# Four waits taken out of GpSimd's tap loop, and its rms step moved up two places

## The reference

```python
# 1. dynamic convolution, 8 heads of 24 features, 7 causal taps, weights by softmax over the taps
w = exp(weight_gen - max(weight_gen)); w = w / (sum(w) + 1e-9)
x1[b, s, h, g] = sum_k w[b, s, h, k] * x_pad[b, s + k, h, g]
# 2. a layer with a rational function, 192 -> 2048 -> 192
h = x1 @ w_in
P = a0 + a1*h + a2*h**2 + a3*h**3
Q = 1 + |b0|*|h| + |b1|*h**2
x2 = (P / (Q + 1e-6)) @ w_out
# 3. RMS norm and a gated layer, 192 -> 1536 -> 192
xn = x2 / sqrt(mean(x2**2) + 1e-6) * rms_g
out = (silu(xn @ w_gate) * (xn @ w_val)) @ w2_out
```

## The kernel before

| step | waits for | VectorE's step, with the iteration's blocks |
|---|---|---|
| mul 2 | `qy_ready` (blk - 2) * 8 + 7 | qy 6 of block i - 2 |
| add 2 | `py_ready` (blk - 2) * 8 + 8 | py 7 of block i - 2 |
| add 3 | `qy_ready` (blk - 1) * 8 + 1 | qy 0 of block i - 1 |
| add 4 | `act_ready` (blk - 1) * 8 + 2 | newton 1 of block i - 1 |

## Time and profile before

### The profile page before, as it was taken

The page is one execution under the profiler, slowest core; times in us unless marked ns, Lnnn a source line. Parts: engine busy times, 40 slices in busy tenths (PEclk is TensorE's granted clock), DMA queues, the critical chain, the costliest instruction groups (busy, mean ns, idle before and its releaser), DMA issues.

```text
span 1418.4 us, 21333 instructions
## 1 busy us (share of the span) xinstructions
PE 1390.6 (98%) x7488; PEld 1248.9 (88%) x7488; DVE 1164.8 (82%) x1520; ACT 1069.3 (75%) x1387; POOL 381.9 (27%) x273
## 2 busy tenths in 40 slices
PE   7879999999999999999999999999999999999998
PEld 6668989989898999889898988989989899898987
DVE  8899978888887888888888788888879788888621
ACT  4877878778788877878887787987878787777521
POOL 3332332404233141332413233240423324000000
PEclk9989999999999999999999999999999999999999
DMA  8201000000000001000000100000000000000000
GB/s 243 77 0 32 2 31 12 15 28 0 31 11 31 11 0 42 0 31 11 31 11 0 42 0 31 11 31 11 0 31 11 31 11 1 12 1 1 12 12 12
DMA packets 12517, 32.35 MB, mean 23 GB/s; under 512 B 1604, under 2 KB 7234, under 8 KB 12480
## 3 DMA queue, kind: packets, MB, share of 16 engines
q1 hardware_dynamic: 11744, 31.61, 6.9%
q10 hardware_dynamic: 736, 0.23, 0.1%
HBM read 25.55 MB, written 6.29 MB: 22 GB/s over the span
## 4 chain that ended last, share of the span: by engine, by line
PE 93%; DVE 4%; ACT 2%; issue 0%; DMA 0%; ACTq 0%; DVEq 0%
PE dn L752 40%; PE bank L743 10%; PE bank L744 10%; PE bank L745 10%; PE bank L746 10%; PE bank L747 10%; PE bank L759 2%; DVE num L681 1%; DVE num L668 1%; PE dn L828 1%; DVE num L665 1%; PE dn L822 1%; DVE den L676 0%; DVE num L687 0%; DVE den L666 0%
## 5 line engine op out<-in xcount | busy, mean ns | idle before, releaser
L752 PE MATMUL dn<-dn_w,num 128*128 128x192 f32 x2048 | 374.9, 327 | 5.4 <-DVE num L687 5.4
L752 PEld LDWEIGHTS dn<-dn_w,num 128*128 128x128 f32 x2048 | 340.5, 191 | 11.7 <-DVE num L687 6.2
L538 ACT ACTIVATE den<-bank,coef 128x512 f32<-128x512 f32 x256 | 175.7, 686 | 177.8 <-PE bank L747 169.8
L752 PE MATMUL dn<-dn_w,glu 128*128 128x192 f32 x1536 | 279.6, 326 | 0.0
L665 DVE TENSOR_TENSOR num<-num,bank 128x512 f32<-128x512 f32 x256 | 174.7, 682 | 111.1 <-ACT num L540 109.2
L752 PEld LDWEIGHTS dn<-dn_w,glu 128*128 128x128 f32 x1536 | 255.0, 190 | 4.0
L681 DVE SCALAR_TENSOR_TENSOR num<-num,coef,seed 128x1024 f32<-128x1024 f32 x128 | 165.9, 1297 | 57.1 <-ACT seed L557 56.6
L540 ACT ACTIVATE num<-bank,coef 128x512 f32<-128x512 f32 x256 | 199.9, 781 | 0.0
L666 DVE SCALAR_TENSOR_TENSOR den<-den,coef,bank 128x512 f32<-128x512 f32 x256 | 189.6, 741 | 0.0
L668 DVE SCALAR_TENSOR_TENSOR num<-num,coef,bank 128x512 f32<-128x512 f32 x256 | 189.6, 741 | 0.0
L712 DVE TENSOR_TENSOR glu<-glu,bank 128x512 f32<-128x512 f32 x192 | 130.8, 681 | 66.2 <-PE bank L747 64.9
(11 more groups left out here) (122 smaller groups left out, 2033.5 us busy)
## 6 DMA issues: line engine op xcount, KB each, us to landing
x_in<-in_x_dram SPq DMA_DIRECT2D x14, 960.0 KB
out_dram<-y_out SPq DMA_DIRECT2D x16, 384.0 KB, 2.3
w_blk<-in_weight_gen_dram SPq DMA_DIRECT2D x14, 112.0 KB, 2.0
dn_w<-in_moe_w_out_dram SPq DMA_DIRECT2D x1, 1536.0 KB, 9.8
dn_w<-in_moe_w_out_dram SPq DMA_DIRECT2D x1, 1152.0 KB, 17.8
num<-in_moe_w_in_dram SPq DMA_DIRECT2D x1, 768.0 KB, 6.3
num<-in_moe_w_in_dram SPq DMA_DIRECT2D x2, 384.0 KB, 7.9
x_in<-in_x_dram SPq DMA_DIRECT2D x1, 768.0 KB
```

The source lines that it names most:

```text
L538: act.activation(chunk(den, c % 8), h, ACT.Abs, scale=B_RAW[:, 1:2])
L752: done = pe.matmul(banks[:, j // 2, j % 2 * D:(j % 2 + 1) * D], acts[:, j * P:(j + 1) * P], w, start=first and j % 2 == 0, stop=last, skip ...
```

## The change

The function `while_reading_psum` and its two calls go, so that `mul 2`, `add 2`, `add 3` and `add 4` start as soon as their data and buffers are there. In GpSimd's program `rms 0 2` moves ahead of `add 3 0` and `mul 5 0`; it stood behind them.

```diff
 POOL_PROGRAM = program("""
-add 6 1, low 4 2, low 5 2, low 6 2, low 7 2, less 0 0, norm 0 0, mul 0 0, mul 1 0, mul 2 0, add 1 0, mul 3 0, add 2 0, mul 4 0, add 3 0, mul 5 0, rms 0 2,
-add 4 0, mul 6 0, add 5 0, low 0 1, low 1 1, low 2 1, low 3 1,
+add 6 1, low 4 2, low 5 2, low 6 2, low 7 2, less 0 0, norm 0 0, mul 0 0, mul 1 0, mul 2 0, add 1 0, mul 3 0, add 2 0, mul 4 0, rms 0 2, add 3 0,
+mul 5 0, add 4 0, mul 6 0, add 5 0, low 0 1, low 1 1, low 2 1, low 3 1,
 """)
...
-            def while_reading_psum(blk, step):
-
-                if step == ("mul", 2):
-                    wait(pool, qy_ready, (blk - 2) * 8 + 7)
-                elif step == ("add", 2):
-                    wait(pool, py_ready, (blk - 2) * 8 + 8)
-                elif step == ("add", 3):
-                    wait(pool, qy_ready, (blk - 1) * 8 + 1)
-                elif step == ("add", 4):
-                    wait(pool, act_ready, (blk - 1) * 8 + 2)
...
                 else:
-                    while_reading_psum(blk, ("mul", k))
                     if k >= 3:
...
             def tap_add(blk, k):
-                while_reading_psum(blk, ("add", k))
                 wait(pool, tap_ready, (blk - 1) * K + k + 1)
```

## The result

The changed kernel takes 1428.57 us (median of 5, 1427.53 to 1430.36), the kernel before 1420.38 us in the same comparison: the ratio is 1.0059, with a 95% interval of 1.0044 to 1.0074. It is slower by 8.2 us. The prediction was 1420.2 us, no change, with 1425.0 as the upper end of its range: it was wrong.

The account below looks back on a forecast made before the run. TensorE, never idle from 105.5 us on, was taken to bound the kernel. VectorE's 2.45 us lateness per iteration came from its own idle, so 0 us over 13 iterations: 1420.2 us forecast, range 1418.0 to 1425.0.

Parts of the forecast that it names:

- What bounds the kernel: TensorE, busy for 1308.50 of 1308.50 us from 105.5 us on, sets the pace; earlier GpSimd steps cannot shorten it.
- the first one of the walk: mul 2 in block 10's iteration: asks at 745.6, waits for two VectorE instructions, ends where the old wait put it; cost 0.
- the walk: Block 10's iteration priced step by step without the waits: VectorE loses about 2.45 us in two places, TensorE 0.
- the row at 116.76: Trace row in an early block: a GpSimd product waited for two L687 in a row, 3.87 us; both kept their time.
- the row at 107.61: Trace row: a GpSimd product met a running L681, took 2.16 us, and got in between two back-to-back L681.
- Both signs of being wrong: TensorE waits for L668, L697 or L712 after 105.5 us; or collisions lengthening more than three VectorE instructions per iteration.
- Rival 2: Two meetings add up ahead of up1 5: 0.41 us per iteration over its slack, 5.3 us slower, 1425.5 us; chance 0.05.
- add 2 and mul 4: Block 10: mul 4 runs 754.9 to 756.4, makes VectorE's L687 1.25 us late; up1 5 keeps 0.65 us; TensorE cost 0.
- rms and add 3: After rms at 776.57, add 3 loses to the first L687; the second ends 1.2 us late; no TensorE cost.
- rival 1: GpSimd wins its turns at 776 to 781: second L687 2.6 us late, up to 7.4 us slower; chance 0.10.
- the threshold of 2.80 us: VectorE lateness allowed at the L697/L665 pair: 2.53 us of idle plus 0.27 us of margin before TensorE loses time.

Follow-up runs that it names:

- The wait removed: The kernel before with only mul 2's wait on qy 6 removed, the other three waits and the old order kept: 1429.13 us, ratio 1.0062.
- the wait put back: The changed kernel with one of its four waits put back, that of mul 2 on qy 6: 1420.87 us, ratio 0.9999.
- the order-alone kernel: The kernel before with only the order changed, rms 0 2 ahead of add 3 and mul 5, all four waits kept: 1420.32 us, ratio 0.9997.
- The closed-pair kernel: The changed kernel with mul 2's wait on qy 6 put back and VectorE's glu 7 moved behind newton 1: 1463.73 us in one run.
- The run with `mul 2` behind `py`: The changed kernel with a wait put back for mul 2, on py 6 in place of qy 6: 1420.34 us, ratio 0.9999.
- the kernel of 1452.9 us: The kernel before with the waits of add 2, add 3 and add 4 removed, mul 2's wait and the old order kept: ratio 1.0233.

## Why the prediction was wrong

*What bounds the kernel* was right: TensorE sets the pace, no GpSimd step was on its path, and nothing was to be gained. Every kernel that was not slower came out within 0.1% of the one before.

*The step that failed* is the first one of the walk: "`mul 2` asks at 745.6, meets a running instruction and another behind it, as at 116.76, and comes out where the old wait had put it. Cost 0." In its place the runs show that `mul 2` goes straight on from `mul 1` and `py 6` waits, that `add 1` then gets in ahead of `qy 6`, and that VectorE loses 3.0 us, not 0. Even in iteration 3, where `mul 2` does wait for `py 6`, it gets in ahead of `qy 6`. The wait removed and the wait put back each move the whole of it. I had taken the row at 116.76, the only one of three in which GpSimd came off worst, for the rule, although the row at 107.61 showed GpSimd between two back-to-back steps. Where three rows disagree, each order should have been priced. (That product also ended 1.40 us behind the second L687, at 120.63 against 119.23, and not 1.54; nothing hangs on it.) Both signs of being wrong that the prediction named are there: TensorE waits for L712's result, and four VectorE instructions per iteration are lengthened, not at most three.

*The margin was not the one I looked at.* Rival 2 had the place and the first loss right ("if `mul 2` gets in ahead of the L681"), but it counted one collision of the two, 0.8 us of lateness, and asked only `up1 5` (1.93 us). The waiter that decided is `down2 2`: 752.89 - 751.25 = 1.64 us behind `glu 2`. With 2.2 us of lateness the excess is 0.6 us, and TensorE lost 0.61 + 0.10. Rival 2 had been given a chance of 0.05.

*add 2 and mul 4*: in the changed kernel they run ahead of `newton 6`, which keeps 1.2 us, because VectorE is late by then. With mul 2 held back (the kernel of 1420.87 us) `newton 6` takes 2.44 us against the 2.5 foreseen, and is covered, as foreseen.

*rms and add 3*: the order was rival 1's and not the walk's: `add 3` gets in ahead of `newton 0`, and `newton 1` is late by 2.4 us where rival 1 had 2.6. That this costs nothing was right, and the order-alone kernel shows it. But the threshold of 2.80 us at the next L665 was not the first one: `gate 9` waits for the `glu 7` between the newton steps. In the kernel before it starts at 780.33, with `glu 7` at 777.91 for 0.68 us, a margin of 1.74; the lateness there is 1.66. The closed-pair kernel, which puts `glu 7` behind a second held-up step, pays 43 us for missing it.

*The Trainium skill's rule* (SBUF — State Buffer, "Who interferes with whom": the first to issue holds the shared ports, the other blocks fully) did better than my reading of 116.76: by it `add 3` beats `newton 0`, which every trace with `add 3` right behind `rms` shows (2.88 us). The run with `mul 2` behind `py` agrees too. At `py 6`, where the time was lost, the trace goes against it: `py 6` started at 751.03, while `mul 1` was still running, `mul 2` 0.04 us later, and `mul 2` went ahead.

*What stays open*: why the product at 116.8 us, and the one at that place in ten of the twelve kernels here, waits for two newton steps. It is not its form, not that it is a product, and not the closed pair. It changed no time.

## What to carry to other kernels

A slack that pays for lateness is the smallest margin of any waiter between the place of the loss and the place where the engine idles again: list the margins of all of them, product by product, before calling a loss covered, and read them in the trace without the stall. Where two engines exclude each other and the rows disagree on who wins, price both orders at each meeting, and carry the lateness on from one meeting to the next. A wait that passes no data may still be the one that matters: here one of four held 8 us, and the other three held nothing with the order changed, but 33 us in the old order with `mul 2` held back.

## What the runs showed of the hardware

- Two engines that want SBUF in this way alternate: `py 6`, `add 1`, `qy 6`, `mul 3` each waited for the one before (2.66, 2.82, 2.86 and 2.40 us instead of 1.28, 1.83, 1.22 and 1.54). A collision breeds the next, since it sets both engines to ask while the other runs.
- Who wins can hang on 0.02 us. In the kernel of 1452.9 us `add 4` asks just ahead of `qy 1`. At 793.42 (`qy 1` at 793.48) GpSimd waited for two steps of VectorE; at 705.59 (`qy 1` at 705.66), in another iteration of the same loop, GpSimd went ahead. In all 13 iterations a lead of 0.05 us lost (four times) and one of 0.07 or 0.08 us won (nine times):

```profile
793.42 4.12 POOL L483 TENSOR_TENSOR conv<-conv,prod 128x768 f32<-128x768 f32 x1
```

```profile
705.59 1.85 POOL L483 TENSOR_TENSOR conv<-conv,prod 128x768 f32<-128x768 f32 x1
```

- A short stall of TensorE costs more than its length: 0.10 us more at each restart after some 0.6 us, and after seven of the thirteen idle times of 2.3 us in the closed-pair kernel a stretch of slower matmuls with the granted clock at 0.50 for 3.3 us.
